# Attention and two MLPs on one core: the last tile's squares get a buffer of their own, one output bank is used last, two splits run later, step 1 is reordered

## The reference

```python
scores = q @ k.T / 8, kept where key < 4 (sinks) or 0 <= query - key < 128
x  = softmax(scores) @ v                       # 2 batches, 8 heads, 768 tokens, 64 channels
h  = x @ w_in                                  # 512 -> 1024
u  = h * softmax(h);  ln = (u - mean) / sqrt(var + 1e-6) * g_ln
x2 = ln @ w_out                                # 1024 -> 512
g  = relu(x2 @ w2_in) ** 2                     # 512 -> 2048
out = g @ w2_out                               # 2048 -> 512
```

## Time and profile before

| | us |
|---|---|
| median of 3 runs | 505.30 |
| the 3 runs | 505.66, 503.95, 505.30 |
| the profiled execution, its own time | 503.79 |
| its span, first to last instruction | 502.1 |
| PE busy in it | 484.4 (96%) |
| DVE, ACT, POOL busy | 287.0, 201.1, 95.5 |

### The profile page before, as it was taken

The page is one execution under the profiler, slowest core; times in us unless marked ns, Lnnn a source line. Parts: engine busy times, 40 slices in busy tenths (PEclk is TensorE's granted clock), DMA queues, the critical chain, the costliest instruction groups (busy, mean ns, idle before and its releaser), DMA issues.

```text
span 502.1 us, 7334 instructions
## 1 busy us (share of the span) xinstructions
PE 484.4 (96%) x2644; PEld 393.3 (78%) x2644; DVE 287.0 (57%) x513; ACT 201.1 (40%) x532; POOL 95.5 (19%) x138
## 2 busy tenths in 40 slices
PE   8989989999999999999789999999999999999997
PEld 6667667888778888877678888888888888888885
DVE  4999898888898887865693433332222232232222
ACT  3667546545665655433343322421211232221121
POOL 2555051120022202357970000000000000000000
PEclk9999999999999999999999999999999999999999
DMA  8921343452222211038100000020000002000002
GB/s 247 289 66 44 113 146 80 121 162 62 55 61 75 60 40 35 14 84 290 22 4 0 1 0 1 0 84 0 0 0 0 0 0 85 0 1 0 0 1 84
DMA packets 39717, 29.21 MB, mean 58 GB/s; under 512 B 29256, under 2 KB 29256, under 8 KB 39176
## 3 DMA queue, kind: packets, MB, share of 16 engines
q1 hardware_dynamic: 39384, 28.56, 19.6%
q10 hardware_dynamic: 304, 0.27, 0.2%
HBM read 22.52 MB, written 3.15 MB: 51 GB/s over the span
## 4 chain that ended last, share of the span: by engine, by line
PE 76%; DVE 14%; SPq 5%; ACT 2%; issue 2%; POOL 1%; DMA 0%; DVEq 0%; POOLq 0%; ACTq 0%
PE score_ps L1407 24%; PE h_ps L1419 12%; PE h_ps L1214 9%; PE w_ps L1252 7%; PE wt_ps L1419 6%; PE w_ps L1419 6%; SPq L342 4%; PE o_ps L1184 2%; PE score_ps L1156 2%; PE wt_ps L1164 1%; DVE prob L905 1%; PE wt_ps L1156 1%; DVE bstat L862 1%; SPq L399 1%; DVE u L855 1%
## 5 line engine op out<-in xcount | busy, mean ns | idle before, releaser
L1407 PE MATMUL score_ps<-x2T_hi,w2in_hi 128*128 (+1 forms) x192 | 74.8, 389 | 0.0
L1407 PE MATMUL score_ps<-x2T_hi,w2in_lo 128*128 (+1 forms) x192 | 74.7, 389 | 0.0
L1407 PE MATMUL score_ps<-x2T_lo,w2in_hi 128*128 (+1 forms) x192 | 74.7, 389 | 0.0
L1089 DVE TENSOR_TENSOR sq<-relu 128x512 f32<-128x512 f32 x24 | 18.6, 775 | 83.2 <-ACT relu L775 83.2
L1089 DVE TENSOR_TENSOR e<-e 128x512 f32<-128x512 f32 x24 | 18.5, 770 | 79.6 <-ACT e L775 79.6
L775 ACT ACTIVATE relu<-score_ps 128x512 f32<-128x512 f32 x24 | 14.4, 598 | 100.0 <-PE score_ps L1407 100.0
L775 ACT ACTIVATE e<-score_ps 128x512 f32<-128x512 f32 x24 | 14.4, 599 | 90.4 <-PE score_ps L1407 90.4
L1407 PEld LDWEIGHTS score_ps<-x2T_hi,w2in_lo 128*128 128x128 f32 x192 | 36.1, 188 | 7.5
L1407 PEld LDWEIGHTS score_ps<-x2T_hi,w2in_hi 128*128 128x128 f32 x192 | 36.0, 188 | 7.5
L1407 PEld LDWEIGHTS score_ps<-x2T_lo,w2in_hi 128*128 128x128 f32 x192 | 36.0, 188 | 7.3
L600 ACT ACTIVATE prob<-sm,nbias 128x132 f32<-128x132 f32 (+1 forms) x96 | 37.8, 396 | 0.5
(11 more groups left out here) (177 smaller groups left out, 1094.8 us busy)
## 6 DMA issues: line engine op xcount, KB each, us to landing
w2in<-w_in SPq DMA_DIRECT2D x4, 1024.0 KB, 5.1
w2out<-w_out SPq DMA_DIRECT2D x8, 512.0 KB, 7.4
V<-v SPq DMA_DIRECT2D x12, 256.0 KB, 2.7
x2T<-x SPq DMA_DIRECT2D x192, 16.0 KB, 1.8
k_raw<-kT SPq DMA_DIRECT2D x20, 132.0 KB, 2.8
q_raw<-qT SPq DMA_DIRECT2D x20, 128.0 KB, 2.8
w2in<-w_in SPq DMA_DIRECT2D x4, 512.0 KB, 6.5
w2in<-w_out SPq DMA_DIRECT2D x2, 1024.0 KB, 11.7
```

The source lines that it names most:

```text
L1089: nc.vector.tensor_tensor(sq[f % 2], relu[f % 2], relu[f % 2], ALU.mult).then_inc(sq_ready, 1)
L1407: done = mm(h2_ps[f % 2], ws[:, c, fs], xs[:, c, bass.ts(blk, BLK)], start=(c == 0 and i == 0), stop=(c == MC - 1 and i == 2))
```

## The change

Five edits. (1) Tile 11's squares go into `y[3]`, a buffer that stage B uses only later, so `square_x2(11)` no longer waits for tile 10's DMAs. (2) `w1_ps` becomes the last of the four output banks, and PE waits for the last squares only in front of that bank's first product instead of in front of all of stage B. (3) The splits of `x2T` blocks 1 and 2 move from f = 2 and 4 to f = 7 and 11. (4) Step 1 is reordered on PE and DVE, and POOL waits for tile 2's normalised row before it builds the second batch's sink values. (5) The two loads of tile 1's q are issued by ACT instead of SP.

```diff
+X2T_AT = (7, 11)
...
-        y_ps = [w0_ps, w1_ps[:, :], h_ps[:, 0:BANK], h_ps[:, BANK:2 * BANK]]
+        y_ps = [w0_ps, h_ps[:, 0:BANK], h_ps[:, BANK:2 * BANK], w1_ps[:, :]]
...
+        def squares_of(t):
+
+            return y[3] if t == NT - 1 else x2[:, :]
+
...
             def move_x2(t):

                 sp.wait_ge(x2_squared, t + 1)
-                squares = x2[:, :].rearrange("p (c r b) -> p c r b", r=QUADS, b=SQ)
+                squares = squares_of(t).rearrange("p (c r b) -> p c r b", r=QUADS, b=SQ)
...
             load_k01(1)
-            for half in range(2):
-                load_q01(sp, 1, half)
             load_w_in(2)
...
         def side_loads(act):
-            for half in range(2):
-                load_q01(act, 0, half)
+            for n in range(2):
+                for half in range(2):
+                    load_q01(act, n, half)
...
                 if t == 2:
+                    pool.wait_ge(ln_ready, 2 * t + 2)
                     build_v_sink(1)
                     split_v_sink(1)
...
-                if f in (2, 4):
-                    round_x2T(f // 2)
+                if f in X2T_AT:
+                    round_x2T(X2T_AT.index(f) + 1)
...
             def square_x2(t):

                 dve.wait_ge(x2_done, t + 1)
-                if t:
+                if 0 < t < NT - 1:
                     dve.wait_ge(x2T_moved[(t - 1) // TB], (t - 1) % TB * MOVES + MOVES)
-                nc.vector.transpose(x2[:, :], x2_ps[:, :]).then_inc(x2_squared, 1)
+                nc.vector.transpose(squares_of(t), x2_ps[:, :]).then_inc(x2_squared, 1)
...
                 row_max(3, 0)
+                split_q(4)
                 square_x2(0)
...
                 split_k(4)
-                split_q(4)
+                normalize_p(3, 1)
                 hidden_max(2, 0)
                 hidden_max(2, 1)
                 hidden_max_all(2)
-                normalize_p(3, 1)
                 gate_and_norm(2)
...
-                if f in (2, 4):
-                    split_x2T(f // 2)
+                if f in X2T_AT:
+                    split_x2T(X2T_AT.index(f) + 1)
...
-                hidden(2, 16, 20)
                 score(3, 2)
                 score(3, 3)
+                hidden(2, 16, 20)
+                transpose_ln(1)
                 hidden(2, 20, 24)
-                transpose_ln(1)
                 project(1, 0, 16)
...
                 for q in range(TB):
+                    if f == 0 and q == TB - 1:
+                        pe.wait_ge(x2_squared, NT)
                     qs = slice(q * P, (q + 1) * P)
...
             hidden2(0, 1, 3, 4)
-            pe.wait_ge(x2_squared, NT)
             with pe.Fori(0, NB - 1) as blk:
```

## The result

The changed kernel takes **498.0 us** (median of four executions, 496.84 to 499.31) against 505.3: a ratio of 0.986, 95% interval 0.983 to 0.989. The forecast was 499.0, faster, with a range of 497.0 to 502.5. The profiled execution takes 498.49 us, its span 496.8: 5.3 less than before in both, where the sum said 5.65. Of all executions in this study one, with edit 2 alone, took 1688.68 us, over three times any other; it is left out of every median and interval.

The account below looks back on a forecast made before the run. PE's own list was taken as the bound, busy 484.4 of 502.1 us, leaving 17.7 idle. 503.79 - 3.65 - 1.6 + 0.3 - 0.7 = 498.14, with 0.9 for the runs' level 499.0 us; range 497.0 to 502.5.

Parts of the forecast that it names:

- the sum: Whole kernel: 503.79 - 3.65 - 1.6 + 0.3 - 0.7 = 498.14 us for an execution like the profiled one.
- Last squares: Turn to stage B: 3.65 us gained; nine products cover the squares with 1.8 us to spare.
- Rival 4: Turn to stage B: the wait only moves behind nine products, 3.65 not had; 501.8 or 502.7 us, chance 0.04.
- Late splits: Stage B, three pairs from 241.04 to 259.03: 1.6 us gained by moving the late x2T splits.
- Chain without slack: Stage B, DVE's chain beside POOL: 0.1 us charged for each of three f, 0.3 lost; ends 0 and 0.9.
- Rivals 2 and 3: Stage B's first block: DVE and POOL hold each other up; rival 2 loses 0.8 a pair, 501.0 or 501.9, chance 0.11.
- Rival 3: Same place, each DVE operation waits out a whole POOL operation: pairs 2.4 late, 507.4 or 508.3 us, chance 0.03.
- Step 1: Step 1 into step 2: 0.7 us gained, SP's queue next limit, queries at 71.5; ends 0.3 lost, 2.8 gained.
- Edit 5: Kernel start: gain 0, ends 0 and 0.5 lost if the first scores fall back toward 6.0 us.
- The 0.9 for executions above the profiled one: Whole kernel: mean of four executions, 504.7, lies 0.9 us above the profiled one; added to the sum.

Follow-up runs that it names:

- edit 2 alone: Kernel before with only w1_ps as last bank and PE's wait in front of it, squares still in the one buffer: 501.21 us, 0.993.
- second run: The changed kernel again, not a line changed: 497.27 us, 0.984 of the kernel before.
- edit 4 alone: Kernel before with only step 1's new order on PE and DVE and POOL's wait: 504.74 us, 0.998.
- first run: The changed kernel with all five edits, as first measured against the kernel before: 498.0 us, 0.986.
- with the queries ahead of the squares: Changed kernel with tile 5's q loads ahead of move_x2(0) on SP's queue: 496.84 us with edit 5 undone, 496.53 with it kept.
- filling the stall: Kernel before with 13 extra products, their result overwritten, ahead of PE's wait at the turn: 503.46 us, 0.996; kernel before beside it 505.63.
- edits 1 and 2: Kernel before with only the last squares' buffer and the late bank: 499.91 us, 0.989.
- edit 1 alone: Kernel before with only the last squares in their own buffer, PE's wait still in front of all of stage B: 499.60 us, 0.989.
- without POOL's wait: Kernel with tile 5's q ahead of move_x2(0) and edit 5 undone, now without POOL's wait for tile 2's normalised row: 497.84 us, 0.987.

## Why the prediction was right, and where it was not

That the first profile's 5.3 us lie so near the sum's 5.65 is in part luck: step 1 gave nothing there (the last `hidden2` product came 0.16 later than before, with the late start in it), the stall 3.70, and stage B up to the fifth pair 1.78, where the sum had 0.7, 3.65 and 1.3. Point by point, with the second run of the changed kernel, whose start agrees with the execution before:

- **Last squares, 3.65 us forecast.** 3.92 between the last `hidden2` product and the first output product became 0.23: 3.69. All by the step as written, the cover of nine products and 1.8 us to spare included. Rival 4 fell. Its price was too high by its own nine products: with edit 2 alone, where the squares do wait for the DMAs, PE waited 1.36 in front of the bank, not the whole stall.
- **Late splits, 1.6.** Three pairs took 17.99; now the pairs stand 5.44 to 5.47 apart, 16.4 for three: 1.6. Right.
- **Chain without slack, 0.3 lost.** Mis-sized: DVE's operations beside POOL are as slow as forecast (`w2out_lo` 1.78, `g_lo` 0.98 in the first run), but of the expected 0.1 a pair 0.03 in all is lost in the first run and nothing in the second. `w2out_lo` of f = 2, done at 248.10, was due at 237.50 + 48 × 0.227 = 248.40: 0.3 to spare where I had read 0.06. The reading was off in two ways. PE began f = 2 at 252.05 before, not at the 251.94 that I had worked out, since its first products behind the stall stood wider apart (the first two 0.33 us), so there were 0.17 to spare. And counted from the first output product the chain now ends after 10.60 us instead of 10.84: `relu` releases it 0.13 earlier, and the square takes 1.61 instead of 1.72. Rivals 2 and 3 fell with it. (Rival 3 would outweigh the gains of 5.95 from 1.5 us a pair on, with four pairs, not from 1.9.) What bounds the chain shows when POOL's rows are laid beside DVE's (first run):

```profile
245.93 1.62 POOL L567 TENSOR_TENSOR w2in_lo<-w2in,w2in_hi 128x512 fp32r<-128x512 f32 x1
247.50 1.07 POOL L565 CAST w2in_hi<-w2in 128x512 fp32r<-128x512 f32 x1
```

`w2out_lo`, started at 246.32, ends at 248.10, 0.55 behind the end (247.55) of the POOL operation that ran when it started. The squares, `g_lo` and `w2out_lo` that start beside POOL's work in stage B all end 0.53 to 0.56 behind such an end, in the first and the second run, so the price of one is the rest of the running POOL operation and not a whole one for each, as rival 3 had it. The Trainium skill, page "SBUF — State Buffer", section "SBUF: two separate sides", has the second of two such operations blocked until the first has ended, and these rows agree.
- **Step 1, 0.7.** 0.74 with edit 4 alone and 1.03 (237.12 less 236.09) in the second run. The limit was the one named, SP's queue: queries at 71.18 to 71.54 where 71.5 was forecast, leaving out the first run with its late start, and with the queries ahead of the squares `project(2)` began at 72.90. The 71.5 itself was luck: the squares' DMAs did begin 0.3 later (57.16 and 57.17 instead of 56.88), but took 10.67 and 10.57 instead of 10.94, so the queries were issued as early as before (67.87 and 67.78 against 67.86), and used by ACT from 71.49 and 71.18 on. The wait for POOL's mask, 0.66 to 0.69 us in these runs, stood in no list of mine.
- **Edit 5, 0.** Not contradicted. The first profile of the changed kernel spoke for a loss of 0.74, beyond my upper bound of 0.5; the repeats showed scatter that neither side of my bounds knew of. The Trainium skill, page "DMA: Bandwidth & Descriptors", section "Issuing engines are not separate DMA queues", by which only issue time is saved, agrees: 496.53 with and 496.84 without.
- **The 0.9 for executions above the profiled one** was the step that failed, and it made the forecast too high by about its own size. I took the level of the runs above the profiled one for a property of the measurement that would stay. For the most part it belongs to the stall: 48 of 49 executions before have a mean clock below 0.998, filling the stall brought it to 0.999 or 1.00 in ten of ten and took 2.2 us off the median, and with edits 1 and 2 all five executions have a mean clock of 0.999 or 1.00, and their median gained 5.6 where the span gained 3.8. The sum without the 0.9, 498.14, lies 0.1 us above the changed kernel's first median and 0.9 above its second. The Trainium skill, page "TensorE: Matmul & The Clock Gate", section "Loop structure matters more than you think", says that PE's clock drops when it waits long for a DMA; two traces agree (0.50 in a wait of 3.41 and of 4.09 us), and the one that I had does not, where 3.53 us of idleness left the clock at 1.00.

In that second run 1.03, 3.69 and 1.67 (three pairs in 16.32) make 6.4 of the 6.6 us by which its span is shorter. Another 0.14 lies in the fourth pair, 5.58 before and 5.44 now: behind a wait PE's first products stand wider apart, so that a wait costs a little more than its idle time. From there the next sixteen pairs take 5.44 each in both.

## What to carry to other kernels

Before pricing a stall from one profiled execution, set the mean granted clock of every execution beside its time: the stall can cost a second time, through PE's clock, in executions that were not profiled, and the one that was profiled can be the exception. A gain ahead of a wait counts only as far as the end of that wait moves too: in the one profile of edit 4 alone, 0.74 us of gain came out as 0.18 behind the wait at the turn. And profile the same kernel twice before a loss at its start is put down to an edit.

## What the hardware showed that I had not expected

- The same idleness of PE at the same place leaves the clock at 1.00 in one execution (3.53 us) and brings it to 0.50 in others (3.41 and 4.09); where the wait was 0.83 us (filled), 0.41 (edit 1 alone) or 1.36 (edit 2 alone), every execution's mean clock was 0.999 or 1.00. So the spread with edit 2 alone (500.10 to 502.41) has another cause, which stays open. A fall without that stall is rare but occurs: one execution of the changed kernel has a mean of 0.996 and takes 499.31, the slowest of its nine, and one without POOL's wait has 0.997 and 499.56, the slowest of its four; where in them the clock fell no trace shows.
- The landing of the first keys moves the first scores: from 7.12 to 5.87 us in two executions of one kernel, and between 5.69 and 6.53 over ten kernels with the same loads. Later waits swallow part of it: 1.25 late there was 0.74 at `project_0`. Kernels with the same instructions up to the turn came there between 236.37 and 237.29, so a difference of half a microsecond between two profiles needs a common starting point before it is read, and the first scores alone are not one: with 5.87 there, `project_0` stood at 54.30 to 54.81.
